# Second mixture of a fused kernel: tiles of 32 tokens on quarters of the array instead of tiles of 128

## The reference

```python
skip_score = x @ w_skip
do_compute = skip_score > 0
...
xc = x[do_compute]
logits = xc @ w_gate
e_idx = np.argmax(logits, axis=1)
...
for e in range(E):
    mask = e_idx == e
    ...
    h = np.maximum(xc[mask] @ w1[e], 0.0)
    y[mask] = gate_w[mask, None] * (h @ w2[e])
out[do_compute] = xc + y
```

## Time and profile before

| | |
|---|---|
| device time, 3 runs | 785.82 us median (785.61 to 786.11) |
| profiled execution, its own time | 785.83 us |
| its span, first to last instruction | 784.1 us |
| PE / DVE / ACT / POOL busy | 96% / 45% / 33% / 10% |
| second mixture, first product to the end of the span | 638.1 to 784.1 us |

### The profile page before, as it was taken

One profiled execution on the slowest core, in us unless ns is written; L12 is line 12 of the kernel. 1 busy time (PEld: TensorE's weight loads), 2 busy tenths in 40 slices (PEclk: granted clock), 3 DMA queues, 4 the chain that ended last, 5 costly groups with the idle time before them and its releaser, 6 DMA issues.

```text
span 784.1 us, 12799 instructions
## 1 busy us (share of the span) xinstructions
PE 753.4 (96%) x4516; PEld 662.8 (85%) x4517; DVE 350.2 (45%) x818; ACT 261.2 (33%) x572; POOL 76.8 (10%) x119
## 2 busy tenths in 40 slices
PE   4699999999999999999999999999999979999996
PEld 4498898989898998989989899898989757788885
DVE  4977573532342121333212143223232579972982
ACT  3754562532230110312102032120202238753862
POOL 2610000000000000000000000001010134231231
PEclk9899999999999999999999999999999989999999
DMA  9992821212330000032000022120203357981830
GB/s 201 202 221 60 170 60 30 49 25 108 108 108 1 1 0 0 0 121 94 0 0 0 0 71 90 54 81 1 81 8 128 112 189 254 392 292 65 294 144 17
DMA packets 77483, 75.05 MB, mean 96 GB/s; under 512 B 54644, under 2 KB 54900, under 8 KB 77056
## 3 DMA queue, kind: packets, MB, share of 16 engines
q1 hardware_dynamic: 74224, 69.82, 29.6%
q0 software_dynamic: 3216, 4.66, 1.9%
HBM read 68.30 MB, written 9.29 MB: 99 GB/s over the span
## 4 chain that ended last, share of the span: by engine, by line
PE 90%; DVE 4%; ACT 2%; DMA 2%; issue 1%; ACTq 0%; POOL 0%; DVEq 0%; SPq 0%; POOLq 0%
PE ps L1195 23%; PE ps L1197 22%; PE ps L1196 22%; PE ps L1490 2%; PE ps L1494 2%; PE ps L1499 2%; PE ps L1468 2%; PE ps L1460 2%; PE ps L1475 2%; PE ps L1229 1%; PE ps L1257 1%; PE ps L1380 1%; PE ps L1449 1%; PE ps L1243 1%; DMA acc<-in_moe_w 1%
## 5 line engine op out<-in xcount | busy, mean ns | idle before, releaser
L666 ACT ACTIVATE h_hi<-ps 128x384 fp32r<-128x384 f32 x128 | 63.0, 492 | 359.0 <-PE ps L1197 359.0
L1195 PE MATMUL ps<-xt_hi,w_hi 128*128 128x384 f32 (+1 forms) x508 | 172.8, 340 | 0.0
L1197 PE MATMUL ps<-xt_hi,w_lo 128*128 128x384 f32 (+1 forms) x508 | 170.0, 335 | 0.0
L1196 PE MATMUL ps<-xt_lo,w_hi 128*128 128x384 f32 (+1 forms) x508 | 169.9, 334 | 0.0
L1195 PE MATMUL ps<-w_hi,h_hi 128*128 128x512 f32 x384 | 151.8, 395 | 0.0
L1197 PE MATMUL ps<-w_hi,h_lo 128*128 128x512 f32 x384 | 149.9, 390 | 0.0
L1196 PE MATMUL ps<-w_lo,h_hi 128*128 128x512 f32 x384 | 149.8, 390 | 0.0
L902 DVE SCALAR_TENSOR_TENSOR h_lo<-ps,h_hi 128x384 fp32r<-128x384 f32 x128 | 71.2, 556 | 168.1 <-ACT h_hi L666 168.0
L1195 PEld LDWEIGHTS ps<-xt_hi,w_hi 128*128 128x128 f32 x508 | 95.4, 188 | 1.5 <-issue 0.8
L1196 PEld LDWEIGHTS ps<-xt_lo,w_hi 128*128 128x128 f32 x508 | 95.5, 188 | 0.5
L1197 PEld LDWEIGHTS ps<-xt_hi,w_lo 128*128 128x128 f32 x508 | 95.3, 188 | 0.0
(11 more groups left out here) (187 smaller groups left out, 805.8 us busy)
## 6 DMA issues: line engine op xcount, KB each, us to landing
stage<-in_moe_w SPq DMA_DIRECT2D x56, 512.0 KB, 4.9
acc<-in_moe_w SPq DMA_DIRECT2D x36, 512.0 KB, 5.8
stage<-in_k SPq DMA_DIRECT2D x16, 192.0 KB, 4.5
acc<-in_v SPq DMA_DIRECT2D x4, 768.0 KB, 6.3
x_rows<-acc SPq DMA_DIRECT2D x4, 768.0 KB, 3.6
out_rows<-acc SPq DMA_DIRECT2D x4, 768.0 KB, 5.2
acc<-in_moe_w POOLq DMA_DIRECT2D x4, 512.0 KB, 4.3
v_all<-in_v SPq DMA_DIRECT2D x16, 120.0 KB, 3.6
```

Of the source, the lines that this page charges most:

```text
L666: nc.scalar.activation(h_hi[:, f, :], ps[:, f % 2, 0:GT], ACT.Relu).then_inc(h_hi_ok, 1)
L1195: mm(dst, a_hi, b_hi, start=start, stop=False)
L1196: mm(dst, a_hi, b_lo, start=False, stop=False)
L1197: return mm(dst, a_lo, b_hi, start=False, stop=stop)
```

## The change

Only the second mixture and what leads into it are changed. A tile has 32 rows (QT), and TILES becomes (1536 + 8 x 31) / 32 = 55. A row of 512 values is spread as four quarters of 128 over four times 32 partitions, so that one gather fills 128 x 128 values and one transposition turns them. Products take plain float32 numbers, without upper and lower parts, so the splits of rows, of hidden values and of weights are gone. In each product 32 columns are loaded into a quarter of the array, and four products that stand one after the other go to the four quarters and write four ranges of 32 partitions: `layer1` has 16 products of 256 moving columns, `layer2` 32 products of 128.

Weights are always multiplied out of one place, `wset[:, 0]`, which lies where `w1_hi` and `w1_lo` were. Three more places lie in the memory of the first mixture's other buffers. SP reads the sets of the experts into them (`load_set`), from the moment that memory is free, and ACT and DVE copy a set into the first place when the expert changes (`place`): 2 pieces of w1 on each, and of w2 3 on DVE and 1 on ACT. The list of rows is read back by ACT instead of SP, four times, and row numbers are made on DVE (`make_ids`) instead of POOL. Loops of DVE and POOL hold 12 tiles in a pass, those of PE and ACT one.

```diff
-    TILES = (N + E2 * (P - 1)) // P
-    SLOTS = 4
+    QT = P // 4
+    TILES = (N + E2 * (QT - 1)) // QT
+    SLOTS = 6
+    AHEAD = 3
+    W1_DVE, W2_DVE = 2, 3
...
+        LAYER = KC * F
+        sets = sb("sets", [P, 2 * KC * F + 2 * ITERS * S + 2 * FC * D + 2 * FC * GT])
+        wset = sets[:, 0:2 * LAYER * (1 + AHEAD)].rearrange("p (s c) -> p s c", s=1 + AHEAD)
...
-        xg = [a1[:, k * D:(k + 1) * D] for k in range(SLOTS)]
+        xg = [a1[:, k * DQ:(k + 1) * DQ] for k in range(SLOTS)]
...
+            def load_set(e, layer):
+
+                for c in range(PIECES):
+                    dst = wset[:, slot_of(e), (PIECES * layer + c) * PIECE:(PIECES * layer + c + 1) * PIECE]
+                    src = w2_piece(v2[e], c) if layer else w1_piece(v1[e], c)
+                    sp.dma_start(two(dst) if layer else dst, src).then_inc(set_in[slot_of(e)][layer], 16)
...
+            sp.wait_ge(l1_done, FC * G * E1)
+            load_set(0, 0)
+            load_set(0, 1)
+            load_set(1, 0)
             store(G - 1)
+            load_set(1, 1)
+            load_set(2, 0)
+            sp.wait_ge(l2_done, GR * G * E1)
+            load_set(2, 1)
+            load_set(3, 0)
+            load_set(3, 1)
...
+            for e in range(1, E2):
+                arrived(e, 1)
+                if e + AHEAD < E2:
+                    sp.wait_ge(w1_by_dve, W1_DVE * (e + 1))
+                    sp.wait_ge(w1_by_act, (PIECES - W1_DVE) * (e + 1))
+                    load_set(e + AHEAD, 0)
+                if e + 1 < E2:
+                    arrived(e + 1, 0)
+                if e + AHEAD < E2:
+                    sp.wait_ge(w2_by_dve, W2_DVE * (e + 1))
+                    sp.wait_ge(w2_by_act, (PIECES - W2_DVE) * (e + 1))
+                    load_set(e + AHEAD, 1)
...
+                nc.gpsimd.indirect_dma_start(xg[k], None, x1_parts, bass.IndirectOffsetOnAxis(of, 0),
...
+            for i in range(1, SLOTS - 1):
+                gp.wait_ge(id_ok, i)
+                gather_rows(i, ids(i))
...
                     with gp.If(i < tiles):
+                        gp.wait_ge(y_ok, i + 2)
                         gp.wait_ge(scattered, 16 * i)
                         hold(gp, "pool")
+                        scatter_rows(at % SLOTS, ids(at))
+                        gp.wait_ge(id_ok, i + SLOTS - 1)
+                        hold(gp, "pool")
+                        gather_rows((at + SLOTS - 1) % SLOTS, ids(at + SLOTS - 1))
...
+            act.wait_ge(x1_kept, 16 * (G - 1))
+            act.wait_ge(entries_out, 16 * NT)
+            for j in range(4):
+                act.dma_start(lst[j * QT:(j + 1) * QT, :, :].rearrange("p c e -> p (c e)"), route_list.rearrange("(p c) e -> p (c e)", p=QT)).then_inc(list_in, 16)
...
+            def relu_h(i):
+                act.wait_ge(r1_done, i + 1)
+                nc.scalar.activation(h2, ps[:, 0, 0:FQ], ACT.Relu).then_inc(relu_ok, 1)
+            def copy_ht(i):
+                act.wait_ge(ht_done, i + 1)
+                nc.scalar.activation(ht2, ps[:, 1, 0:FQ], ACT.Copy).then_inc(ht_ok, 1)
+            def place(then, at, layer):
+                act.wait_ge(set_ready, 2 * then + 1 + layer)
+                for c in range(W2_DVE if layer else W1_DVE, PIECES):
+                    cols = slice((PIECES * layer + c) * PIECE, (PIECES * layer + c + 1) * PIECE)
+                    nc.scalar.activation(wset[:, 0, cols], wset[:, bass.ds(at, 1), cols].rearrange("p o c -> p (o c)"),
+                                         ACT.Copy).then_inc(w2_by_act if layer else w1_by_act, 1)
...
             with act.Fori(1, TILES) as i:
                 with act.If(i < tiles):
+                    now, then = set_at(i), set_at(i + 1)
                     with act.If(now < then):
+                        at = waiting_at(i + 1)
+                        place(then, at, 0)
+                        copy_ht(i)
+                        relu_h(i + 1)
+                        act.wait_ge(r2_done, i + 1)
+                        place(then, at, 1)
                     with act.Else():
+                        copy_ht(i)
+                        relu_h(i + 1)
...
+            def copy_x(i):
+                dve.wait_ge(x_tr, i + 1)
+                nc.vector.tensor_copy(xt2, ps[:, 4, 0:P]).then_inc(x_ok, 1)
...
+            def make_ids(i, k):
+                col = dve.value_load(table[0:1, bass.ds(i + COL_OF, 1)], min_val=0, max_val=COLS - 1)
+                nc.vector.tensor_scalar(id_of[:, k % TURNS:k % TURNS + 1], lst[:, bass.ds(col, 1), 0], quarter[:, 0:1], None, ALU.add).then_inc(id_ok, 1)
+            def add_x(i, k, col):
+                dve.wait_ge(r2_done, i + 1)
+                nc.vector.scalar_tensor_tensor(out=xg[k % SLOTS], in0=ps[:, 2, 0:DQ], scalar=lst[:, bass.ds(col, 1), 1], in1=xg[k % SLOTS],
                                                op0=ALU.mult, op1=ALU.add).then_inc(y_ok, 1)
+            def rows_in(k, uses):
+                dve.wait_ge(gathered[k % SLOTS], 16 * uses)
+                nc.vector.tensor_copy(x_in, xg[k % SLOTS]).then_inc(rows_ok, 1)
+            def place(i, then, layer):
+                at = dve.value_load(table[0:1, bass.ds(i + 1 + PLACE_OF, 1)], min_val=0, max_val=AHEAD)
+                dve.wait_ge(r2_done if layer else r1_done, i + 1)
+                dve.wait_ge(set_ready, 2 * then + 1 + layer)
+                for c in range(W2_DVE if layer else W1_DVE):
+                    cols = slice((PIECES * layer + c) * PIECE, (PIECES * layer + c + 1) * PIECE)
+                    nc.vector.tensor_copy(wset[:, 0, cols], wset[:, bass.ds(at, 1), cols].rearrange("p o c -> p (o c)")).then_inc(
+                        w2_by_dve if layer else w1_by_dve, 1)
+
+            tiles = dve.value_load(table[0:1, 0:1], min_val=1, max_val=TILES)
+            dve.wait_ge(list_in, 16 * 4)
+            for i in range(1, SLOTS + 1):
+                make_ids(i, i)
+            now, then = set_at(0), set_at(1)
             with dve.If(now < then):
-                low_ht(0, 1)
-                lows_w1(then, range(PIECES // 2))
-                low_x(1)
-            with dve.Else():
+                place(0, then, 0)
+            dve.wait_ge(r2_done, 1)
...
+            with dve.If(now < then):
+                place(0, then, 1)
+            copy_x(1)
+            copy_x(2)
+            rows_in(3, 1)
...
+                    i, at = TURNS * r + k + 1, k + 1
                     with dve.If(i < tiles):
+                        col = dve.value_load(table[0:1, bass.ds(i + COL_OF, 1)], min_val=0, max_val=COLS - 1)
+                        copy_x(i + 2)
+                        rows_in(at + 3, 2 * r + 1 + (at + 3) // SLOTS)
+                        now, then = set_at(i + 1), set_at(i + 2)
+                            place(i + 1, then, 0)
+                        add_x(i, at, col)
+                        now, then = set_at(i), set_at(i + 1)
+                        with dve.If(now < then):
+                            place(i, then, 1)
+                        make_ids(i + SLOTS, at + SLOTS)
+                        if k + 1 < TURNS:
                             turn(k + 1)
...
+            def layer1(i, now):
+
+                pe.wait_ge(x_ok, i + 1)
+                    if c < W1_DVE:
+                    for j in range(4):
+                        at = c * F + j * FQ
+                        last = mm(ps[j * QT:(j + 1) * QT, 0, 0:FQ], xt2[:, c * QT:(c + 1) * QT], wset[:, 0, at:at + FQ],
+                                  start=(c == 0), stop=(c == KC - 1))
+                last.then_inc(r1_done, 1)
+
+            def turn_h(i):
...
+            def layer2(i, now):
+
+                pe.wait_ge(ht_ok, i + 1)
+                pe.wait_ge(y_ok, i + 1)
+                for f in range(FC):
...
+                    at = f % (FQ // P) * P + f // (FQ // P) * QT
+                    for j in range(4):
+                        to = LAYER + f * D + j * DQ
+                        last = mm(ps[j * QT:(j + 1) * QT, 2, 0:DQ], ht2[:, at:at + QT], wset[:, 0, to:to + DQ],
+                                  start=(f == 0), stop=(f == FC - 1))
+                last.then_inc(r2_done, 1)
...
-            tile(0, 0, 0, nothing, lambda: transpose_x(1, 1), first=True)
+            turn_h(0)
+            layer2(0, 0)
+            with pe.Fori(1, TILES) as i:
+
+                with pe.If(i < tiles):
+                    layer1(i + 1, set_at(i + 1))
+                    pe.wait_ge(rows_ok, i)
+                    transpose_x(x_in)
+                    layer2(i, set_at(i))
+                    turn_h(i + 1)
```

More of the change, by code:

```diff
@@ L434, in _ @@
+            sp.wait_ge(table_ok, 1)
+            tiles = sp.value_load(table[0:1, 0:1], min_val=1, max_val=TILES)
             sp.wait_ge(scattered, 16 * tiles)
@@ L760, in _ @@
-            split_x(0)
-            for c in range(PIECES // 2, PIECES):
-                split_w2(E1, c, stage2[:, c, :])
-            relu_h(0, 0)
-            act.wait_ge(table_ok, 1)
```

(26 more changed lines are left out.)

427 lines of the change are left out of this document (151 added, 276 removed).

## The result

The changed kernel takes 829.5 us (median of 3, 828.54 to 832.73) where the kernel before takes 785.82: 1.0565 times as long, 95% interval 1.052 to 1.061. Its profiled execution took 828.54, with a span of 826.8. The forecast was 826, in a range of 804 to 866.

The account below looks back on a forecast made before the run. DVE's register work was taken to bound the turns: start to 668.7, 20 turns to 795.7, last tile to 800.3, empty passes and leaving to 824.6, plus 1.7 gives 826 us (5% slower), range 804 to 866.

Parts of the forecast that it names:

- DVE becomes the bound: In plain turns, DVE's loads, tests and short work take 5.4 us a tile, more than PE's 4.7 to 5.3.
- Start: Second mixture's start: list at 646, then row numbers and copies on DVE, tile 1's layer 1 at 658.5, loop at 668.7 us.
- Not late for anyone: At the start, tile 0 begins at about 638 us as before, and no engine waits for it.
- Turns: The 20 loop turns before the last tile's: 12 plain ones 64.8 us, eight with weight changes, together 127.
- End: Last tile done at 800.3 us, then PE's 32 empty passes, 24.0, and 0.3 to leave; POOL's exit ends earlier.
- its own range: Whole kernel, from turns of 4.6 to 6.0, start 655 to 662 and copies at half price: 804 to 848 us.
- Pairs: Rival for PE's products: quarters of the array only pair up, turn some 7 to 8.1 us, +36, 862 us; 13%.
- the issue floor: In layer 2, if 0.038 us between matmuls is a floor for issuing, its 64 short ones take 2.4 us.
- Clock: Rival for plain turns: PE's clock falls to half, 8.2 us a tile; 843 us if half the time, 860 always; 15%.
- Weights not there: Rival for weight transfers: expert 3's set, wanted at 671 us, comes 15 late at the lower rate, 840 us; 7%.
- Register work hides: Rival for DVE's loads: they run beside short data work, turn 4.7 us; with faster empty passes about 772 us; 7%.
- Jumps: Rival for DVE's new loop: jumps cost more, one delay of 1 us a turn makes 20 more, 846 us; 10%.

Follow-up runs that it names:

- the run with the early signal: Changed kernel with SP signalling that expert 0's weights are there before it issues the last 16 transfers of the start, not after: 830.0 us.
- The run with four loads: Changed kernel with a table column telling whether a tile begins a new expert, so DVE loads four numbers a plain turn instead of six: 821.19 us.
- the weights in place: Changed kernel without weight copies: expert e multiplied from place e mod 4, PE code written out by expert, two DVE loads a turn, no empty passes: 814.63 us.
- the three together: Changed kernel with PE and ACT loops ending at the last tile, four DVE loads instead of six, and DVE's jump back announced: 803.85 us.
- the last version with weights in place: As the weights in place, but expert 4's weights asked for after tile 1's first layer instead of tile 0's, and DVE's jump back announced: 799.33 us.

## Why the prediction was right, point by point

**The main mechanism held, one step of it did not.** The products became cheaper, and the kernel slower through work that is no arithmetic: a start without work, changes of expert, empty passes. But "DVE becomes the bound" is not borne out in the plain turns. By the prediction's own signs the turn there should be 5.4 and PE's gaps should end with DVE's copy; it is 4.86, and PE's one gap of 0.4 ends with its own load. That the sum came out only 2 us low in the span (824.6 forecast, 826.8 measured) is partly luck, with errors that cancel.

**Start.** Forecast 658.5 for tile 1's layer 1, measured 660.5. Two terms were mis-sized in opposite directions. The list was put at 646, between 643.4 and 647; it came at 650.0, outside my bounds, for I had bounded only its reading back by one weight transfer. The last pairs of the list landed 5.3 us after issue (637.4 to 642.7), and only then were the four reads issued, which took up to 5.9. A copied piece was put at 1.0; five took 3.2, 0.64 each. The estimate from the Trainium skill ("VectorE: DVE Perf Modes", "Mode 2×_2P — use both read ports for one tensor"), which has two elements a cycle for such a copy, was nearer 0.6: here the trace agrees, with 0.71 busy for one (L1176) and starts 0.61 apart. Tile 0 did not begin at 638 but at 650.2, behind SP's last transfers. "Not late for anyone" held, as the run with the early signal shows.

**Turns.** 20 turns were put at 127 and took 126.9 (from copy L1126 at 671.0 to 797.95), which is luck. The 12 plain ones took 62.8 against 64.8, of which 3.0 are DVE's jump back that the forecast did not have. Without it a turn is 4.98 where I took 5.4, and 4.86 once the turn behind a change is past. DVE's own row of work I had put at 4.6 if all data work hides beside the loads, and it nearly does, so it fits beside PE's chain of 4.86, which lies inside my 4.7 to 5.3. The run with four loads decides between the two: the pace stays, so it is PE's. Its 0.4 at the loop's head, the load of the next expert, I had not priced. The eight turns with changes took 64.2 against 62.1.

**End.** The last tile was put at 4.6 and took 5.75 (797.95 to 803.7): when its copy came, PE was still in the layer 2 before. The empty passes were put at 24.3 and took 22.8 (803.7 to 826.5). Without them 11 us go, not 24: POOL's exit stands behind them, 6.2 us where I took 4.07, and is over 11 us after the last product; the forecast named it as hidden, and the run shows where it ends.

**Range.** The bounds of "its own range", 804 to 848, do not come out of the terms named there: all three low terms give 798.5, the two high ones 841.5. The measured time lies inside either.

**Rivals.** *Pairs:* four quarters do run at once; layer 2's 1.95 lies between my 1.8 and the issue floor 2.4. The price of pairs was 52, not 36: a plain turn goes to 7.9, inside the rival's 7 to 8.1, but from 4.86 and not from 5.4. *Clock:* 1.00 in plain turns, with PE at 92%; below that only behind the waits of the start and of changes. *Weights not there:* they were; a signal for them was late. *Register work hides:* in plain turns it does, nearly; 4.86 is closer to this rival's 4.7 than to my 5.4. At the start, in turns with changes and in empty passes it does not: there each load with its steps costs 0.6 and more. *Jumps:* this had more in it than its 20 us were argued from. In the changed kernel one shows, 3.0 us on DVE; but jumps ate part of the gain of the weights in place. The Trainium skill ("Runtime: NRT & Kernel Launch", "Instruction fetch mechanics") describes a taken branch to what has not been fetched as a wait for a transfer. The runs agree: the jumps took 6.4 and 5.1 us with weights on the queues and 4.9 and 3.2 with fewer, each with a transfer of code in it; PE's own short jump back took 0.2, and DVE's wait was gone once its jump was announced.

Of the 43.7 us lost, the runs place 25: 11 in the empty passes, 8 in two of DVE's six loads, some 3 in its jump back (by the trace; no time of a run shows it alone), and the rest of the 25 shows only with the three together. The other 18 were not taken apart, though the last version with weights in place, without copies, takes back 30 in all. The trace has them at the start, where tile 1's layer 1 begins 22 us after the kernel before began with products (660.5 against 638.1) with one tile done between, and in the eight turns with changes, 8.0 each against 4.86, less what the cheaper products give back.

## What to carry to other kernels

Smaller tiles divide the arithmetic and multiply everything that is paid for once a tile: count a turn's register loads, tests and jumps on each engine (here 0.6 to 0.7 us a load) beside its products, and see which chain is the longest: in plain turns six loads on DVE just fitted beside PE's chain and cost nothing. A loop to the greatest possible count costs its empty passes once nothing else ends later; give it the real count. A long wait in a list of waits is worth only what follows it: PE's 10 us for SP were worth 0, while two loads a turn on an engine that hardly shows as busy were worth 8, all of them where the expert changes and PE waits for that engine. A shorter wait can also pay twice: behind 6.2 us of idle PE went on at half clock, behind 3.4 at full.

## What the runs showed of the hardware

An instruction that issues a transfer took up to 3.1 us on SP's queue while earlier ones were in flight (0.47 in the median), so a signal that SP gave at 631.4 ahead of sixteen of them came at 650.1 behind them, and tile 0 began 9 us later. A jump forward over code that is not run cost up to 6.4 us on PE, of which 3.8 passed before the transfer of the code began. On one chip of three the same layer 2 took 2.2 to 3.8 instead of 1.95 us in plain turns, its weight loads idle between matmuls, while the kernel before, with its longer matmuls, ran at 786.1 there as elsewhere; why stays open.
